# Gated-tile low parts moved from GpSimd to VectorE, a new table of down pieces, and w_out split during the first attention

## The reference

```python
scores = np.where((rel >= 0) & (rel < 64), scale * q @ k.T, -1e9)
x = softmax(scores) @ v                       # per head, heads side by side: (4, 576, 512)

h = np.maximum(x @ w_in, 0.0)                 # (4, 576, 1024)
conv_out = sum(conv_w[k] * hp[:, k:k + S] for k in range(3))
x2 = h * sigmoid(conv_out) @ w_out            # (4, 576, 512)

h = np.maximum(x2 @ w_in2, 0.0)
u, v = h[..., :512], h[..., 512:]
v_n = (v - mean) / sqrt(var + 1e-6)
v_s = einsum('ts,bsd->btd', w_spatial, v_n) + b_spatial
out = (u * v_s) @ w_out2
```

## Time and profile before

| | before |
|---|---|
| median of 3 runs | 560.69 us (559.03 to 561.02) |
| profiled execution, its own time | 560.64 us |
| its span, first to last instruction | 558.8 us |
| busy in the span: PE, DVE, ACT, POOL | 508.1, 274.0, 249.7, 160.6 us |
| mean granted TensorE clock | 0.969 |

### The profile page before, as it was taken

How to read it: one execution, slowest core, us unless ns; L and a number is a source line. 1 busy time by engine, 2 the same in 40 slices (tenths; PEclk the granted TensorE clock), 3 DMA queues, 4 the chain that set the end, 5 groups by cost and what they waited for, 6 DMA issues and landing times.

```text
span 558.8 us, 10566 instructions
## 1 busy us (share of the span) xinstructions
PE 508.1 (91%) x4432; PEld 474.5 (85%) x4432; DVE 274.0 (49%) x487; ACT 249.7 (45%) x638; POOL 160.6 (29%) x155
## 2 busy tenths in 40 slices
PE   5779569999779999499999999899999999999997
PEld 3579558899668999398999898897999799989997
DVE  3869944627926539636459715363304330432020
ACT  4828553517745338635268517325311531153111
POOL 3654632202422204322114214134203420342030
PEclk9989869999979999889999999899999999999999
DMA  8880000260001430002540100000100010001002
GB/s 271 268 330 2 0 1 21 77 245 2 0 1 48 156 139 1 0 2 78 190 143 1 38 1 1 1 1 1 65 22 1 0 65 22 0 1 73 14 0 86
DMA packets 15586, 33.09 MB, mean 59 GB/s; under 512 B 1330, under 2 KB 4402, under 8 KB 14772
## 3 DMA queue, kind: packets, MB, share of 16 engines
q1 hardware_dynamic: 13284, 28.22, 14.7%
q10 hardware_dynamic: 2256, 4.21, 2.2%
HBM read 27.71 MB, written 4.72 MB: 58 GB/s over the span
## 4 chain that ended last, share of the span: by engine, by line
PE 64%; DVE 22%; ACT 8%; DMA 2%; issue 2%; POOL 1%; SPq 0%; ACTq 0%; DVEq 0%
PE dense L354 43%; PE dense L539 11%; DVE tmp L817 10%; DVE tmp L828 5%; PE x_ps L401 3%; DVE qk L900 3%; PE pt_ps L388 3%; ACT vp L594 2%; PE score L375 2%; DMA x2keep<-w_in 2%; PE score L369 1%; DVE negmax L768 1%; POOL vrstd L1035 1%; ACT tmp L626 1%; DVE wr L823 1%
## 5 line engine op out<-in xcount | busy, mean ns | idle before, releaser
L354 PE MATMUL dense<-ar,wr 128*128 128x288 f32 x1152 | 170.4, 305 | 11.1 <-POOL ar L1000 7.0
L354 PEld LDWEIGHTS dense<-ar,wr 128*128 128x128 f32 x1152 | 161.0, 195 | 14.7 <-issue 8.3
L354 PE MATMUL dense<-xr,wr 128*128 128x288 f32 x1152 | 158.1, 298 | 2.6 <-ACT tmp L723 2.1
L354 PEld LDWEIGHTS dense<-xr,wr 128*128 128x128 f32 x1152 | 155.8, 191 | 3.6 <-ACT tmp L723 2.4
L817 DVE SCALAR_TENSOR_TENSOR tmp<-tmp,taps 128x576 f32<-128x576 f32 x64 | 68.6, 1072 | 23.7 <-ACT tmp L626 22.5
L1000 POOL TENSOR_TENSOR ar<-tmp,ar 128x576 fp32r<-128x576 f32 x32 | 42.9, 1346 | 107.0 <-ACT ar L637 107.0
L988 POOL TENSOR_TENSOR vp<-vp,recip 128x512 f32<-128x512 f32 x36 | 37.5, 1042 | 92.3 <-DVE recip L793 92.3
L594 ACT ACTIVATE vp<-score,bias 128x128 f32<-128x128 f32 x128 | 45.3, 366 | 35.5 <-DVE bias L772 34.9
L539 PE MATMUL dense<-wr,ar 128*128 128x288 f32 x448 | 60.2, 295 | 0.0
L539 PEld LDWEIGHTS dense<-wr,ar 128*128 128x128 f32 x448 | 59.7, 188 | 0.0
L1048 POOL TENSOR_TENSOR ar<-vp,ar 128x576 fp32r<-128x576 f32 x16 | 24.6, 1539 | 119.6 <-ACT ar L733 119.6
(11 more groups left out here) (76 smaller groups left out, 516.0 us busy)
## 6 DMA issues: line engine op xcount, KB each, us to landing
vp<-v_rows SPq DMA_DIRECT2D x36, 256.0 KB, 3.0
out_t<-vp SPq DMA_DIRECT2D x16, 288.0 KB, 2.1
qk<-k_t SPq DMA_DIRECT2D x3, 1152.0 KB, 5.4
qk<-q_t SPq DMA_DIRECT2D x3, 1152.0 KB, 7.8
x2keep<-w_in ACTq DMA_DIRECT2D x2, 1024.0 KB, 7.4
qk<-w_in SPq DMA_DIRECT2D x1, 2048.0 KB, 9.2
x2keep<-w_out ACTq DMA_DIRECT2D x1, 1280.0 KB, 7.4
vp<-w_spatial_t SPq DMA_DIRECT2D x1, 1152.0 KB
```

The source lines that it names most:

```text
L354: last = mm(dst, stationary(a, t), moving(c, t), start=(t == 0 and n == 0), stop=(t == (of or len(tiles)) - 1 and n == 2))
```

## The change

It has three parts. The low part of each gated tile (32 in all) is subtracted on DVE as the third item of its loop (`up` runs one iteration longer, and the subtraction is for tile f-2); POOL has nothing to do in `up` any more. `SHARES` becomes 24 pieces after step 0, then 4 or 3. The splitting of `w_out` moves into the first attention: all high parts go to ACT in steps 10, 11 and 12, the low parts of pieces 0 to 2 stay on DVE, those of 3 to 7 on POOL before the first `up`, and the DMA of the last 3 tiles is issued in step 11 in place of after step 12.

```diff
-        SHARES = [5, 10, 5, 5, 4, 4, 5, 5, 5, 6, 5, 5]
+        SHARES = [24, 4, 4, 4, 4, 4, 4, 4, 3, 3, 3, 3]
...
-            act.wait_ge(trans_done, NB)
-            act.dma_start(raw_out_b, w_out_t[:, OUT_A:FT, :]).then_inc(out_loaded[1], 16)
+                if t == STEPS - 2:
+                    act.wait_ge(trans_done, NB)
+                    act.dma_start(raw_out_b, w_out_t[:, OUT_A:FT, :]).then_inc(out_loaded[1], 16)
+                for i in {STEPS - 3: (0, 1), STEPS - 2: (2, 3), STEPS - 1: (4, 5, 6, 7)}.get(t, ()):
+                    act.wait_ge(out_loaded[0 if i < OUT_A else 1], 16)
+                    nc.scalar.activation(wout[0][:, i, :], raw_out(i), ACT.Copy).then_inc(split_hi_out, 1)
...
-            def up(b, pieces=()):
-                for f in range(FT + 1):
+            def up(b):
+                for f in range(FT + 2):
...
-                    for i in pieces[f:f + 1]:
-                        dve.wait_ge(out_loaded[0 if i < OUT_A else 1], 16)
-                        vec.tensor_copy(wout[0][:, i, :], raw_out(i)).then_inc(split_hi_out, 1)
-                    if f >= 1:
+                    if 1 <= f <= FT:
...
+                    if f >= 2:
+                        e = f - 2
+                        dve.wait_ge(gated_hi, FT * b + e + 1)
+                        vec.tensor_tensor(gated[1][:, e, :], conv[:, e % 4, :], gated[0][:, e, :].bitcast(F32),
+                                          ALU.subtract).then_inc(gated_lo, 1)
...
-                    vec.tensor_copy(wout[0][:, i, :], raw_out(i)).then_inc(split_hi_out, 1)
...
-            def up(b, pieces=()):
-                for f in range(FT):
-                    for i in pieces[f:f + 1]:
-                        pool.wait_ge(split_hi_out, i + 1)
-                        pl.tensor_tensor(wout[1][:, i, :], raw_out(i), wout[0][:, i, :].bitcast(F32),
-                                         ALU.subtract).then_inc(split_lo_out, 1)
-                    pool.wait_ge(gated_hi, FT * b + f + 1)
-                    pl.tensor_tensor(gated[1][:, f, :], conv[:, f % 4, :], gated[0][:, f, :].bitcast(F32),
-                                     ALU.subtract).then_inc(gated_lo, 1)
...
-            up(0, range(OUT_FIRST, N_PIECES))
+            for i in range(OUT_FIRST, N_PIECES):
+                pool.wait_ge(split_hi_out, i + 1)
+                pl.tensor_tensor(wout[1][:, i, :], raw_out(i), wout[0][:, i, :].bitcast(F32),
+                                 ALU.subtract).then_inc(split_lo_out, 1)
             for b in range(0, B - 1):
                 for j in range(NB):
                     normalise(j, NB * b + NB + j)
-                up(b + 1)
```

More of the change, by code:

```diff
@@ L841, in _ @@
                 i = t - (STEPS - OUT_FIRST)
-                if i == 0:
-                    dve.wait_ge(out_loaded[0], 16)
                 if i >= 0:
-                    vec.tensor_copy(wout[0][:, i, :], raw_out(i)).then_inc(split_hi_out, 1)
                     dve.wait_ge(split_hi_out, i + 1)
@@ L852, in _ @@
             dve.wait_ge(zero_cols, 1)
-            up(0, range(OUT_FIRST, N_PIECES))
+            up(0)
             for b in range(0, B - 1):
```

## The result

The changed kernel takes 534.88 us (median of 4 runs, 532.13 to 535.96), the kernel before, measured beside it, 560.85 us. The ratio is 0.9553, 95% interval 0.9521 to 0.9584. The forecast was 531.4 us, within 526 to 541. The profiled execution takes 535.08 us with a span of 533.2 us, 25.6 less than before.

What follows compares the result with a forecast made beforehand. PE was taken as the bound, busy 508.1 of 558.8 us, with a 7.22 us wait for exponentials. Terms -14.0 (later rounds), -12.5 (first round), -1.6 (first attention), -1.1 (last batch) sum to -29.2: 531.4 us from 560.64, range 526 to 541.

Steps and rivals of the forecast that it cites:

- T - S: From the start of window 0's scores (S) to that of window 1's (T): 11.5 us, +0.9 against 10.60.
- V - T: From the start of window 1's scores (T) to the next up (V): 34.4 us against 42.27, -7.9.
- the first round: First stretch from window 0's scores to the next up: 15.93 and 42.53 us become 11.5 and 34.4, -12.5.
- The block of 72 matmuls: PE's work placed ahead of window 1's scores: 9.6 us, starting at 227.4 after a 0.5 us cost.
- steps 1 to 3: Steps after window 1's scores start: less PE work than the softmax chain, whose 3.37 us sets each step.
- DVE in up: Low part on DVE at 0.75 us, 3.1 us a tile against PE's 3.2: up stays 25.63 us, zero gain.
- The first attention: Start to first scores: w_out DMA taken as 5.6 us, ReLU at 42.0, -1.6 us; bounds -3.2 and +1.2.
- ACT waiting for `w_out` to 42 us: Sign in the first attention that would show the forecast wrong; the last w_out DMA was to land before 40 us.
- The last batch: PE's 1.27 us wait for low part 6 goes; the third block's first conversions come earlier: -1.1 us.
- A: Rival: the clock sinks in steps 1 to 3 through PE idleness; +14 us, 545 us; chance 0.07.
- B: Rival: DVE becomes the bound of up, low part costing 1.22 us; +13 and +3, 547 us; chance 0.06.
- C: Rival: the 72-matmul block runs at 1.2 GHz, 18.9 us in place of 9.6; 568 us; chance 0.04.

Runs made afterwards that it cites:

- shares_only: The kernel before with nothing but the new SHARES table: 538.33 us, ratio 0.9617 to the kernel before.
- old_shares: The changed kernel with the old SHARES table put back: 555.45 us, ratio 0.9923 to the kernel before.
- block12: The changed kernel with SHARES starting at 12 pieces in place of 24, the rest spread over later steps: 545.87 us, ratio 0.9781 to the kernel before.
- low_on_pool: The changed kernel with the low part of the gated tiles back on POOL, new SHARES and w_out splitting kept: 535.20 us, ratio 0.9558.
- low_dve_only: The kernel before with nothing but the low part of the gated tiles moved to DVE: 555.50 us, ratio 0.9925.
- late_dma: The changed kernel with the DMA of the last three w_out tiles issued in step 12 again: 535.00 us, ratio 0.9557 to the kernel before.
- qk_behind_wout: The changed kernel with SP's load of the next q and k waiting until the last w_out tiles have landed: 529.64 us, ratio 0.9466.
- casts_in_up: The changed kernel with ACT's last three w_out casts moved behind sigmoids of the first up: 530.62 us, ratio 0.9477 to the kernel before.
- early4: The changed kernel with the casts moved as in casts_in_up, EARLY 4 in place of 5, and SHARES refilled: 524.40 us, ratio 0.9373.
- all_three: The changed kernel with q and k loads delayed as in qk_behind_wout, plus the EARLY and SHARES of early4: 521.94 us, ratio 0.9359.

## Why the prediction was right, and where it was off

**The rounds.** The forecast's main terms hold within 0.4 us each: T - S 11.5, measured 11.38; V - T 34.4, measured 34.42; the first round -12.5, measured -12.7. The block of 72 matmuls took 9.78 us (forecast 9.6), ACT's exponentials were ready when PE reached T, and steps 1 to 3 took the 3.37 us of the softmax chain. That the wait was filled, and not shortened, is shown by `shares_only`, `old_shares` and `block12`. Two small things in the working were off. Its own terms, 227.4 + 9.6, give 237.0 for PE's arrival at T and not 237.2. And it had the exponentials hold T at 11.2 us behind S; they hold it at 10.66 (`old_shares`), mostly since DVE's bias takes 0.17 us in place of 0.55 with POOL idle. The margin was 0.7 us, not 0.3.

**DVE in up.** The low part at 0.75 us was right (0.753), and `up` stayed at 25.63 us. The forecast gave this part no gain in the rounds, which `low_on_pool` confirms. The account of the first round blamed the `w_out` casts, slowed by POOL, for the 5.75 us wait. Moving the low part alone left 5.91 us (`low_dve_only`); moving the `w_out` splitting alone, with the new table, left 0.86 (`low_on_pool` against 5.75 in `shares_only`). So it was the splitting of `w_out`. Its DVE casts and POOL's low parts of it went together, and how much was due to which was not tried.

**The first attention: wrong.** The step that failed is "I take 5.6 since loads of q and k are under way, which gives a ReLU at 42.0": the DMA took 9.0 us, the ReLU was done at 44.5, and the term was +3.3 in place of -1.6, outside its own bounds of -3.2 and +1.2. I had priced the DMA by its duration, and for that the trace before had the right answer in another form: the landing at 42.2 was not an issue time plus 5.3, it was the time at which the engines had finished everything in flight (in the trace before they moved 403 GB/s from 40 to 41 us, 137 in the next, then none). The prediction had named ACT waiting for `w_out` to 42 us as a sign of being wrong, and that sign came. `late_dma` (issued 1.7 us later, landed at the same time) and `qk_behind_wout` (4.5 us without the other loads) settle it. The rule of the Trainium skill ("Trainium Kernel Development and Optimization", Key Constraints) that the prediction set against its own number, that DMAs from different queues run on the same 16 engines and interleave, agrees with these runs: 9.0, 7.2 and 4.5 us for the same 768 KB. The late ReLU is 2.6 of the 4.9 us. The other 2.3 are the clock: behind the 4.4 us wait 144 matmuls took 21.59 us, 2.25 more than in `qk_behind_wout`. The forecast had no such term. The time stayed inside the range because that range is 15 us wide and the other terms made up 1.4 us. For this term that is luck: its own bounds did not hold.

**The last batch** gained 1.8 where 1.1 was forecast. The 1.27 us wait went, and so did the small ones around it: 192 matmuls now run in 25.44 us without a wait.

**The rivals.** A (clock sinking in steps 1 to 3): PEclk is 1.00 over 77.48 to 111.90 with waits of 0.44 to 0.84 us in it. The Trainium skill ("TensorE: Matmul & The Clock Gate", A second HAM failure mode: psum-queue depth-cycling) spoke for this rival, and the traces here do not bear it out for such waits. The rival's first argument misread a row: the 0.89 is the mean of the stretch that holds the 7.22 us wait, not of one after it. B (DVE the bound of `up`): 25.63 us says no. C (cold block, slower than before): the block ran at 1.00 behind its 0.93 us wait. With longer waits it does cost: 0.85 behind 2.85 us in `casts_in_up`.

## What to carry to other kernels

When PE waits for a chain on other engines and has independent work further back in its queue, the independent work placed in front of the wait can be worth more than a faster chain (here about 21 us, against 4.4 for the low part alone): measure the wait, divide by the price of a piece, and stop where the chain is ready. A DMA's landing is to be read as an instant, together with what else is on the engines; before moving an issue earlier, ask what it shares them with, and whether the other load could go second. An instruction that waits for a DMA should not stand in an in-order queue ahead of one that PE needs.

## What the runs showed of the hardware that I had not expected

The granted clock had fallen behind PE waits of 2.85 us (0.85 over the next 11.25 us), 4.0 us (0.96 over 38.81), 4.4 us (0.88 over 21.52) and 7.2 us; behind waits of 0.93 and 1.27 us it had not. Between them the same kernel code came out both ways. Behind the 1.7 us wait in the first attention the clock was 0.52 over the next 2 us in the kernel before and 1.00 in `shares_only`, worth 1.2 us. Behind the 2.1 us wait in the third block 48 matmuls took 8.1 to 8.2 us in eight of the twelve traces (clock 0.79 in the changed kernel) and 6.63 us in the other four (`old_shares`, `casts_in_up`, `early4`, `all_three`; clock 1.00 in `old_shares`). The prediction had put no clock loss behind a wait in the first attention.

DVE and POOL hold each other up. DVE's two taps took 1.67 us alone and 2.69 with POOL's 1.20 us subtraction beside them; where POOL's subtraction and DVE's multiplication of the gated tile overlapped, both grew, DVE from 0.75 to 1.77 us and POOL to 1.55, both from `low_on_pool`:

```profile
194.89 1.55 POOL L992 TENSOR_TENSOR ar<-tmp,ar 128x576 fp32r<-128x576 f32 x1 [18.33 <-ACT ar L637]
195.28 1.77 DVE L829 TENSOR_TENSOR tmp<-tmp 128x576 f32<-128x576 f32 x1
```

A cast on DVE, with one input, was held up as well: 1.51 us in place of 0.42 beside POOL's low parts of `w_out` in the kernel before. Yet the 1.0 us a tile that DVE lost in the later `up` phases was slack, and its removal was worth nothing in the time with the new table.
